# First batch's token columns cast in halves, input quarters one unit sooner, no dummies beside the first units

## The reference

```python
# attention: batch 2, 8 heads, 768 rows, head size 64, first 8 keys global, 96 local
scores = scale * q @ k.T + bias                 # bias = -slope(head) * distance
scores = where(is_global | is_local, scores, -1e9)
a = exp(scores - max) / (sum + 1e-09)
x = (a @ v) as [batch, row, head * 64]          # 2 x 768 x 512

# gated block: d_ff 1024
h = relu(x @ w_in);  u, v = halves of h
v_n = (v - mean) / sqrt(var + 1e-6)
v_s = w_spatial @ v_n + b_spatial
x = (u * v_s) @ w_out

# second block: rank 32, hidden size 2048
u = x + (x.T @ U @ V).T
out = u + relu(u @ w_ch1) @ w_ch2
```

## Time and profile before

| | |
|---|---|
| median of three runs | 531.86 us (531.8 to 532.62) |
| profiled execution, its own time | 531.5 us |
| its span | 529.6 us |
| TensorE busy | 518.2 us (98%) |
| VectorE, ScalarE, GpSimd busy | 278.2, 187.8, 135.9 us |
| mixing steps of the first batch begin | 102.89 us |
| last `probs_v` | 181.29 us |

### The profile page before, as it was taken

One profiled execution on the slowest core, in us unless ns is written; L12 is line 12 of the kernel. 1 busy time (PEld: TensorE's weight loads), 2 busy tenths in 40 slices (PEclk: granted clock), 3 DMA queues, 4 the chain that ended last, 5 costly groups with the idle time before them and its releaser, 6 DMA issues.

```text
span 529.6 us, 7583 instructions
## 1 busy us (share of the span) xinstructions
PE 518.2 (98%) x2654; PEld 407.7 (77%) x2654; DVE 278.2 (53%) x767; ACT 187.8 (35%) x470; POOL 135.9 (26%) x166
## 2 busy tenths in 40 slices
PE   6999999999999999999999999999999999999996
PEld 5666666677777788888888888888888888888885
DVE  5778898797776358775422555241255522111112
ACT  5777777767666433232420101020010121001010
POOL 7853604122222011480599920000000000000000
PEclk9999999999999999999999999999999999999999
DMA  7898756645743023292133300020000002000002
GB/s 159 195 214 152 142 114 137 128 82 104 136 69 111 15 46 52 38 192 48 40 120 119 120 1 2 0 80 0 1 0 0 1 0 81 0 1 0 1 0 84
DMA packets 72186, 36.89 MB, mean 70 GB/s; under 512 B 57424, under 2 KB 66896, under 8 KB 72144
## 3 DMA queue, kind: packets, MB, share of 16 engines
q1 hardware_dynamic: 51024, 20.10, 18.6%
q0 software_dynamic: 4512, 14.29, 9.7%
q10 hardware_dynamic: 16608, 1.97, 2.6%
HBM read 32.15 MB, written 3.15 MB: 67 GB/s over the span
## 4 chain that ended last, share of the span: by engine, by line
PE 86%; DVE 7%; issue 3%; ACT 2%; DMA 1%; DVEq 0%; SPq 0%; ACTq 0%
PE ps L1464 74%; PE ps L1429 4%; PE ps L1485 4%; PE ps L1513 3%; DVE sc L1045 2%; PE ps L1602 1%; ACT pr L695 1%; DMA qk_first<-in_q 1%; DVE q_turned L987 1%; DVE pr L1060 1%; PE ps L1612 1%; DVE xT_lo L1018 0%; DVE small L1117 0%; DVE small L1057 0%; ACT pT L709 0%
## 5 line engine op out<-in xcount | busy, mean ns | idle before, releaser
L1373 DVE SCALAR_TENSOR_TENSOR hT_lo<-ps,hT_hi 128x512 fp32r<-128x512 f32 x48 | 33.2, 692 | 167.5 <-ACT hT_hi L904 167.5
L904 ACT ACTIVATE hT_hi<-ps 128x512 fp32r<-128x512 f32 x48 | 28.7, 598 | 223.2 <-PE ps L1464 223.2
L695 ACT ACTIVATE pr<-sc,small 128x256 f32<-128x256 f32 (+1 forms) x96 | 46.2, 483 | 31.7 <-DVE small L1045 31.5
L1045 DVE CUSTOM_DVE_ANT_0 sc<-ps,bias 128x256 f32<-128x256 f32 (+1 forms) x96 | 35.0, 400 | 10.5 <-PE ps L1485 8.7
L1464 PE MATMUL ps<-win_hi,xT_hi 128*128 128x512 f32 x96 | 39.9, 416 | 0.4 <-issue 0.4
L1214 DVE STREAM_TRANSPOSE ys<-tokens 32x128 f32<-32x128 f32 x128 | 38.6, 302 | 1.8
L1464 PE MATMUL ps<-win_hi,xT_lo 128*128 128x512 f32 x96 | 37.7, 393 | 0.0
L1464 PE MATMUL ps<-win_lo,xT_hi 128*128 128x512 f32 x96 | 37.5, 391 | 0.0
L1464 PE MATMUL ps<-uT_hi,w1a_hi 128*128 128x512 f32 x96 | 37.5, 390 | 0.0
L1464 PE MATMUL ps<-uT_hi,w1a_lo 128*128 128x512 f32 x96 | 37.4, 389 | 0.0
L1464 PE MATMUL ps<-w2a_hi,hT_hi 128*128 128x512 f32 x96 | 37.3, 389 | 0.0
(11 more groups left out here) (161 smaller groups left out, 1114.5 us busy)
## 6 DMA issues: line engine op xcount, KB each, us to landing
w_raw<-in_moe_w_ch POOLq DMA_DIRECT2D x16, 512.0 KB, 4.1
vn<-in_v SPq DMA_DIRECT2D x12, 256.0 KB, 3.7
out<-ys SPq DMA_DIRECT2D x11, 256.0 KB, 2.2
wsp<-in_moe_w_spatial POOLq DMA_DIRECT2D x28, 96.0 KB, 3.4
qk_late<-in_q SPq DMA_DIRECT2D x24, 112.0 KB, 3.8
qk_late<-in_k SPq DMA_DIRECT2D x24, 112.0 KB, 3.6
vp<-in_v SPq DMA_DIRECT2D x10, 224.0 KB, 4.4
w_raw<-in_moe_w_in POOLq DMA_DIRECT2D x4, 512.0 KB, 5.0
```

Of the source, the lines that this page charges most:

```text
L695: act.activation(pr[:, k % 3, e, 0:w], sc[:, k % 2, e, 0:w], ACT.Exp, bias=nmax[:, k % 2, e:e + 1], scale=-1.0, accum_out=sums[:, k % 3, e ...
L904: act.activation(hT[0][:, n % 2, :], h1_ps(n), ACT.Relu).then_inc(s["hT_hi"], 1)
L1045: dve.tensor_tensor_reduce(out=sc[:, k % 2, e, 0:w], in0=scores_ps(k, e)[:, 0:w], in1=bias[:, 2 * p + e, WINDOW - w:WINDOW], scale=-SCALE, ...
L1373: dve.scalar_tensor_tensor(hT[1][:, n % 2, :], h1_ps(n), 0.0, hT[0][:, n % 2, :], ALU.max, ALU.subtract).then_inc(s["hT_lo"], 1)
```

## The change

Three things. The token columns of each tile of the first batch are cast in two halves: columns of pairs 0 and 1 (`x_half_hi`, `x_half_lo`) as soon as their two `probs_v` are done, the rest in `x_hi` and `x_lo`, where the whole was cast. TensorE waits for the first half's subtraction before it writes pair 2 into the same bank. `LAG` becomes 5 and `ALONE` 29: quarter 0 stands behind unit 3, quarters 1, 2 and 3 in units 5, 7 and 8, and from unit 9 on unit k carries quarter k-5; each mixing step begins one unit sooner, and the last one has a fourth unit, 47, right behind 46. The dummies beside units 0 to 3 are gone; the five ahead of the first transposes stay.

```diff
-LAG = 6
+LAG = 5
+QUARTERS = {5: 1, 7: 2, 8: 3}
...
             def x_hi(tile):
                 wait(act, "av", (tile + 1) * NP)
-                act.activation(xT[0][:, :, ...], x_ps(tile)..., ACT.Copy).then_inc(s["xT_hi"], 1)
+                c = slice(CM // 2 if tile < NT else 0, CM)
+                act.activation(xT[0][:, c, ...], x_ps(tile)...[:, c, :], ACT.Copy).then_inc(s["xT_hi"], 1)
+            def x_half_hi(tile):
+                wait(act, "av", tile * NP + NP // 2)
+                act.activation(xT[0][:, 0:CM // 2, ...], x_ps(tile)...[:, 0:CM // 2, :],
+                               ACT.Copy).then_inc(s["x_half_hi"], 1)
...
# ScalarE, in the loop over ALONE, ahead of exps(k + 2)
+                    if k % NP == 3 and k // NP < NT:
+                        x_half_hi(k // NP)
...
# VectorE
+            def x_half_lo(tile):
+                dve.wait_ge(s["x_half_hi"], tile + 1)
+                hi, lo = [w[:, 0:CM // 2, tile * P:(tile + 1) * P] for w in xT]
+                dve.tensor_tensor(lo, x_ps(tile)...[:, 0:CM // 2, :], hi, ALU.subtract).then_inc(s["x_half_lo"], 1)
...
# VectorE, in the loop over ALONE, ahead of unit(k)
+                    if k % NP == 3 and k // NP < NT:
+                        x_half_lo(k // NP)
...
# TensorE, probs_v(k)
+                if tile < NT and p == NP // 2:
+                    pe.wait_ge(s["x_half_lo"], tile + 1)
...
                 def unit(k, between=None):
-                    if k < NP:
-                        keep_busy(k, 2)
                     probs_transpose(k)
...
                         if q == 0:
+                            pe.wait_ge(s["x_half_lo"], t + 1)
+                        if q == 1:
                             wait(pe, "xT_lo", t + 1)
...
-                    unit(k, 0 if k == LAG - 1 else k - LAG if k > LAG else None)
+                    unit(k, QUARTERS.get(k) if k < LAG + NP else k - LAG)
...
+                    if k == 3:
+                        pe.wait_ge(s["chunk_split"], 1)
+                        wait(pe, "biased", 2 * 6)
+                        u_v_piece(0, 0, 0, False)
...
-                    if a + 2 <= LAST:
-                        unit(a + 2)
+                    unit(a + 2)
+                unit(LAST)
                 probs_v(LAST)
```

More of the change, by code:

```diff
@@ L342, in program @@
             piece_hi chunk_hi chunk_split u_split v4_hi v4_split
-            xT_hi xT_lo uv v_done u_relu v_relu stats_ready meanvar_ready var_ready rstd_ready normed
+            x_half_hi x_half_lo xT_hi xT_lo uv v_done u_relu v_relu stats_ready meanvar_ready var_ready rstd_ready normed
             gv_hi gv_split wsp_turned wspT_hi wspT_lo mixed gate gate_transposed gT_hi gT_lo
@@ L684, in x_hi @@
                 wait(act, "av", (tile + 1) * NP)
-                act.activation(xT[0][:, :, tile % NT * P:(tile % NT + 1) * P],
-                               x_ps(tile).rearrange("p (c n) -> p c n", c=CM), ACT.Copy).then_inc(s["xT_hi"], 1)
+                c = slice(CM // 2 if tile < NT else 0, CM)
+                act.activation(xT[0][:, c, tile % NT * P:(tile % NT + 1) * P],
+                               x_ps(tile).rearrange("p (c n) -> p c n", c=CM)[:, c, :],
+                               ACT.Copy).then_inc(s["xT_hi"], 1)
+            def x_half_hi(tile):
+                wait(act, "av", tile * NP + NP // 2)
+                act.activation(xT[0][:, 0:CM // 2, tile * P:(tile + 1) * P],
+                               x_ps(tile).rearrange("p (c n) -> p c n", c=CM)[:, 0:CM // 2, :],
+                               ACT.Copy).then_inc(s["x_half_hi"], 1)
             def exps(k):
@@ L886, in window @@
                         wsp_hi(0, 1, 1, False)
-                    if a + 2 <= LAST:
-                        probs_out(a + 2)
+                    probs_out(a + 2)
+                probs_out(LAST)
                 x_hi(TILES - 1)
@@ L1016, in x_lo @@
                 wait(dve, "xT_hi", tile + 1)
-                hi, lo = [w[:, :, tile % NT * P:(tile % NT + 1) * P] for w in xT]
-                dve.tensor_tensor(lo, x_ps(tile).rearrange("p (c n) -> p c n", c=CM), hi,
+                c = slice(CM // 2 if tile < NT else 0, CM)
+                hi, lo = [w[:, c, tile % NT * P:(tile % NT + 1) * P] for w in xT]
+                dve.tensor_tensor(lo, x_ps(tile).rearrange("p (c n) -> p c n", c=CM)[:, c, :], hi,
                                   ALU.subtract).then_inc(s["xT_lo"], 1)
+            def x_half_lo(tile):
+                dve.wait_ge(s["x_half_hi"], tile + 1)
+                hi, lo = [w[:, 0:CM // 2, tile * P:(tile + 1) * P] for w in xT]
+                dve.tensor_tensor(lo, x_ps(tile).rearrange("p (c n) -> p c n", c=CM)[:, 0:CM // 2, :], hi,
+                                  ALU.subtract).then_inc(s["x_half_lo"], 1)
             def set_bias(tile):
```

## The result

The changed kernel is slower by 3.6 us: 535.69 us (median of 4 runs, 535.33 to 536.09) against 532.13 us for the kernel before beside it (4 runs, 531.8 to 532.62), ratio 1.0068 with a 95% interval of 1.0056 to 1.0080. The forecast was 533.3 with a range of 530.8 to 534.3. Its sign is right, its size is not: the time lies 1.4 us beyond the range. Two mechanisms of the prediction are there at their places; three terms of its sum were too small, and a fourth, costed at nothing, was not nothing.

What follows compares the result with a forecast made beforehand. TensorE, busy 518.2 of 529.6 us, was taken as the bound. Terms 1.41 + 0.25 + 1.2 - 3.3 - 1.0 + 0.2 - 0.2 = -1.4 us put the 531.86 us median at 533.3, range 530.8 to 534.3.

Steps and rivals of the forecast that it cites:

- Dummies: Units 0 to 3: about 3.0 us of calls go, mostly turning into TensorE idle time; the clock's rise stays where it was.
- First half cast: Tile 0, up to unit 7: 0.8 us gained early is spent, a shorter later cast returns some; gain 0.25 us.
- Quarters one unit sooner: From unit 8 on, one quarter more is done at the same unit: six matmuls, 1.41 us gained.
- What LAG moves on VectorE: Units 8 to 27: statistics ahead of biased scores make TensorE stand, 3.3 us lost; old stands of 1.2 us vanish.
- The later half casts: Tiles after the first: 0.1 us more each on VectorE and ScalarE, covered by existing waits, so costed at nothing.
- First mixing step: Stream transposes now precede VectorE's last normed and gv_lo; projection 9.4 us in instead of 8.38, 1.0 us lost.
- Later steps: Mixing steps after the first: a 0.33 us cast wait goes, about 0.2 for scores comes; gain 0.2 us with moved order.
- Last step: Units 46 and 47 back to back: transposes of 47 need ScalarE's copy of 46; 0.2 us lost.
- the quarter is kept: Rival: VectorE absorbs the statistics in spare time, no stands at units 10 to 26; 530.4 to 530.9 us, chance 0.2.
- Cancelled: Rival: the stands come, but the first mixing step loses 0.4 us or less; 531.9 to 532.7 us, chance 0.25.
- The clock's: Rival: without dummies TensorE's clock rises a stretch later, about 1 us on top; 534.3 us, chance 0.12.
- quarter 0 starts no sooner: Rival: the half cast holds quarter 0 at its old start, so 1.41 us is lost too; 534.7 us, chance 0.03.

Runs made afterwards that it cites:

- stats_later: The changed kernel with the layer norm work of VectorE and ScalarE's gv_hi one unit later, where they stood before the change; 532.30 us, ratio 1.0003 to before.
- halves_alone: The kernel before with only the half casts and TensorE's wait for them added; 533.67 us, ratio 1.0033 to before.
- last_step: The changed kernel with unit 46 ahead of the last projection instead of behind it; 535.96 us, ratio 1.0073 to before.
- thirty_ kernels: Three kernels with unit 29 ahead of the first mixing step again, one on the changed kernel, two on stats_later; 535.05, 532.37 and 532.32 us.
- thirty_stats: stats_later with unit 29, without a quarter, ahead of the first mixing step again, so each step is as before; 532.37 us, ratio 1.0015 to before.
- thirty_stats_last: thirty_stats with the first batch's last-tile statistics on VectorE moved behind the biased scores, directly ahead of their normed; 532.32 us, ratio 1.0001 to before.
- dummies_back: The changed kernel with the two dummies beside each of units 0 to 3 again; 535.99 us, ratio 1.0074 to before.
- before_no_dummies: The kernel before with only the dummies beside units 0 to 3 left out; 532.29 us, ratio 1.0005 to before.

## Why the prediction was wrong, point by point

**In short.** By the spans the sum was -1.4 and the result -4.5. Of the 3.1 us between them 0.9 are the first half cast's term, 1.2 the order behind unit 8, 0.8 the last step's. The chain that the prediction followed is the right one; these three terms each left out a wait, named below.

**What bounds.** Right: TensorE's stands grew by 4.0 us. Its busy time grew by 0.5, though 3.0 us of dummies are gone: the long durations lasted until 20.3 in this trace. The kernels without dummies and with an early rise have 515.5 to 516.5 us of busy time, those with a late one 517.8 to 518.7.

**Dummies.** Right that they stand ahead of work that waits: no change either way in two kernels. That the rise stays where it was failed in this trace (past 20.3 and not 16.4), at 0.35 us. The Trainium skill's page "TensorE: Matmul & The Clock Gate", Part 1, has activity release the clock. The traces agree in part, for with dummies the rise is early in all three that were seen (between 16 and 17 us) and without them now early, now late. As a price the rule is small here, 0.35 us.

**First half cast, +0.25, measured -0.65.** This step failed. It had ScalarE's half cast from 19.15 and VectorE's done at 19.85; they were at 19.45 to 19.81 and 20.19, for of the 0.7 us that the first unit gained (11.31 against 12.02) 0.46 were left at unit 2 (its copy began at 19.18, 19.64 before). VectorE and ScalarE in after, where the earlier trace rows stood:

```profile
19.84 0.42 DVE L1036 TENSOR_TENSOR xT_lo<-ps,xT_hi 128x256 fp32r<-128x256 f32 x1 [1.03 <-ACT xT_hi L693]
20.19 0.41 DVE L1063 CUSTOM_DVE_ANT_0 sc<-ps,bias 128x256 f32<-128x256 f32 x1
```

```profile
19.45 0.36 ACT L693 ACTIVATE xT_hi<-ps 128x256 fp32r<-128x256 f32 x1
```

It missed a wait: `probs_v` of unit 2 is held by the half's subtraction. With an early clock that is visible (0.63 us ahead of 20.42 in stats_later), with the late one TensorE comes later than it. Quarter 0 began at 21.74 and not 21.0, and unit 4 at 23.82 and not 22.95. Of the 0.9 us by which unit 8 missed, 0.35 are the clock's by the comparison above; of the rest, 0.4 are there at unit 4 with the early clock (23.35 in stats_later against 22.95), which is this chain, and 0.2 more come by unit 7.

**Quarters one unit sooner, +1.41.** Right: they are in every trace, quarter 3 in unit 8 waited for nothing. Where VectorE's order is that of before, 0.9 of them are left at the first mixing step.

**What LAG moves on VectorE, -3.3 and 1.2 back.** The mechanism is shown: the layer norm a unit later returns 3.4 us of time. The sizes were off. From the pace, units 8 to 10 lose 0.90 us where 0.54 were forecast, 12 to 14 0.53, 16 to 18 0.58, 18 to 20 0.37 where nothing was, 20 to 22 1.14 and 24 to 26 0.98 where 0.7 stood, 26 to 27 0.22 for 0.3: 4.7 in place of 3.3, against which the old stands at units 23 and 27 are gone (0.86), as forecast. Stands 14 and 18 were right to 0.04 us. The others each lack something. At unit 10 it is the keys: the second stream transpose began 1.32 us behind the first, 0.94 before, and 0.38 on top of 0.54 is 0.92. (The longer normalising there, L1078 with 0.70 us, cost nothing: it ended at 41.27, ScalarE's half at 41.35.) At unit 22 the biased scores would have begun at 79.03 without the statistics and began at 80.28; 2.12 on from 79.03 is 81.15, and TensorE would have been ready at 81.26 (75.04 and 6.22 as before), so only 0.11 of the 1.25 us was covered. At unit 19 it is ScalarE, which the prediction left out: its `gv_hi` goes by k minus LAG too, and now stands, with the cast of the low-rank factor (`v_st`, from 69.02), ahead of the exponentials, whose biased scores were done by 69.2:

```profile
69.76 0.62 ACT L756 ACTIVATE gv_hi<-vnf 128x512 fp32r<-128x512 f32 x1
70.27 0.50 ACT L704 ACTIVATE pr<-sc,small 128x256 f32<-128x256 f32 x1
```

**The later half casts, at nothing.** Wrong in halves_alone, which loses 1.3 us for them, mostly at units 20 and 24, where their cover is thin: at unit 20 they stand behind the stream transposes of the spatial weights (`turn_wsp` in unit 18). In stats_later they cost 0.35 us at unit 12 and nothing at units 20 and 24. What they cost in after was not measured apart; the stands at units 10, 14, 18 and 19 are explained without them.

**First mixing step, -1.0, measured -1.01.** The best step: projection at 9.4 in, found at 9.39, by following VectorE's queue entry for entry. Two kernels with the old steps have 8.34 and 8.35. In stats_later, with the same step, it is 9.11.

**Later steps, +0.2, measured +0.1.** Right in kind: the wait of 0.33 us for the cast (at 136.67 before) is gone, and one of 0.37 for scores has come in step 1 (at 125.65), where about 0.2 was counted.

**Last step, -0.2, measured -1.04.** Failed. The sum followed units 46 and 47 (0.19 idle ahead of unit 47, as forecast) and overlooked the wait ahead of the projection: 0.45 for `gT_lo` at 180.07, which with the first products behind it is about 0.75 us. VectorE began `gT_lo` at 176.41 before, having waited for ScalarE. Now it has a tile's cast and the biased scores of unit 47 to do between the gate and `gT_lo` and begins it at 179.33, 0.8 us behind ScalarE's `gT_hi` (done at 178.56), while TensorE's second unit has no scores left to issue. last_step shows that the order isn't what costs it, and the thirty_ kernels that three units don't have it.

**The rivals.** That the quarter is kept fell (the stands came). Cancelled fell by the first mixing step. The clock's came true in the trace at a third of its price; the 0.43 us for a product at the low level stands in no row here, and quarter 0 came behind the rise (0.50 at 21.74, the next five 0.39 to 0.40). That quarter 0 starts no sooner fell: 21.74 against 25.17.

## What to carry to other kernels

Moving work up on the busiest engine by one place shifts whatever else is placed by the same index; list for each engine what then stands ahead of the instruction that the others wait for. Here one index moved 1.27 us of statistics in front of it, and with the rest of the layer norm cost 3.4 us. Earned time was not kept, since the next reader's chain got no shorter: stats_later, thirty_stats and thirty_stats_last have the second batch within 0.2 us of each other (182.32 to 182.51), each with its stand in another spot. And follow the last instance of a repeated step by itself, with the work that it no longer has as cover.

## What was not expected of the hardware

- The rise to TensorE's short durations, without dummies, came by 14.8 us in two executions, between 15.6 and 16.7 in three and between 20.3 and 21.3 in six; with dummies, in three, between 16 and 17. The granted clock reads 1.00 in all of it.
- One set of loads had two lengths, and they go with the dummies. Four issues of `qk_odd` on SyncE took 1.85 or 1.86 us in the three profiled executions with dummies (before, dummies_back, halves_alone) and 2.81 to 3.31 in the eleven without. Before and before_no_dummies differ in nothing else, nor do dummies_back and after. The second stream transpose then waited for the keys in four of the eleven, 1.10 us in before_no_dummies, which lost 0.5 us at unit 10. Why the dummies matter to these issues is open, and the medians show no price. SyncE in before and in before_no_dummies:

```profile
27.71 1.86 SPq L410 DMA_DIRECT2D qk_odd<-in_k  x4
```

```profile
27.70 3.24 SPq L410 DMA_DIRECT2D qk_odd<-in_k  x4
```

- The normalising of 128x256 on VectorE took from 0.35 to 0.72 us with nothing of its own changed. Up to the end of the units the six of before and after that took over 0.6 us all began while a `TENSOR_TENSOR` of GpSimd ran, and ended 0.14 to 0.16 us behind its end, as this one of GpSimd (end 41.11) and the normalising at 40.57 (end 41.27). The reverse doesn't hold throughout: one in each trace that began beside a longer one of GpSimd (`v_st`, 1.19 and 1.20 us) took 0.39. No run takes the GpSimd work away, so this is a coincidence in time and no shown cause:

```profile
40.39 0.72 POOL L524 TENSOR_TENSOR wout_lo<-w_raw,wout_hi 128x256 fp32r<-128x256 f32 x1
```
